# Attention scores of a chunked linear-attention step: two fp32 matmuls of 64 rows in place of three fp32r passes over a block-diagonal operand

## The reference

```python
for t in range(S):
    state = alpha[:, :, t, :, None] * state + np.einsum('bhd,bhe->bhde', k[:, :, t], v[:, :, t])
    y[:, :, t] = np.einsum('bhd,bhde->bhe', q[:, :, t], state)
...
h = np.maximum(xt @ w_tok1, 0.0) @ w_tok2          # token mixer, xt is x transposed
u = x + h.transpose(0, 2, 1)
h2 = np.maximum(u @ w_ch1, 0.0) @ w_ch2            # channel mixer, result u + h2
...
k = np.maximum(xk @ w_k, 0.0); v = k * k @ w_v     # channel mix
r = 1.0 / (1.0 + np.exp(-(xr @ w_r)))              # result r * v
```

## Time and profile before

| quantity | value |
|---|---|
| median of three runs | 812.43 us |
| span of the profiled execution | 811.5 us, 0.9 below the median |
| PE / DVE / ACT / POOL busy | 96% / 61% / 41% / 13% of the span |
| attention of batch 0 alone | 8.4 to 59.1 us |
| three passes of the loop | 59.1 to 471.9 us |
| last mixer and channel mix | 471.9 us to the end |

### The profile page before, as it was taken

How to read it: one execution, slowest core, us unless ns; L and a number is a source line. 1 busy time by engine, 2 the same in 40 slices (tenths; PEclk the granted TensorE clock), 3 DMA queues, 4 the chain that set the end, 5 groups by cost and what they waited for, 6 DMA issues and landing times.

```text
span 811.5 us, 14781 instructions
## 1 busy us (share of the span) xinstructions
PE 779.0 (96%) x4864; PEld 765.0 (94%) x4864; DVE 492.4 (61%) x1463; ACT 332.8 (41%) x848; POOL 103.9 (13%) x146
## 2 busy tenths in 40 slices
PE   6998999999999999899999999999699999999998
PEld 5887999998899999899999999999699999999998
DVE  7987777872677776367787522224835744744751
ACT  4773434331333433143334213125445644743741
POOL 2564000201000110100020013003200000000000
PEclk9999999999999999999999999999899999999999
DMA  9973223330132232112232003200101101101000
GB/s 189 202 171 64 40 42 52 66 57 21 40 51 40 41 69 40 41 30 40 48 50 74 1 30 99 93 30 16 45 29 50 39 29 49 39 29 49 10 29 29
DMA packets 114895, 43.88 MB, mean 54 GB/s; under 512 B 102160, under 2 KB 112016, under 8 KB 114832
## 3 DMA queue, kind: packets, MB, share of 16 engines
q1 hardware_dynamic: 113680, 38.36, 22.8%
q0 software_dynamic: 1152, 4.72, 1.6%
HBM read 33.63 MB, written 9.44 MB: 53 GB/s over the span
## 4 chain that ended last, share of the span: by engine, by line
PE 81%; DVE 8%; issue 5%; ACT 3%; POOL 1%; SPq 1%; DMA 1%; DVEq 0%; ACTq 0%; POOLq 0%
PE bank L633 17%; PE bank L617 17%; PE bank L699 12%; PE bank L677 12%; PE bank L686 5%; PE bank L538 3%; PE bank L522 3%; PE bank L597 3%; PE bank L500 2%; PE bank L603 2%; PE bank L541 2%; PE bank L571 2%; PE bank L544 1%; ACT qs_hi L756 1%; DVE decay L893 1%
## 5 line engine op out<-in xcount | busy, mean ns | idle before, releaser
L756 ACT ACTIVATE qs_hi<-qd,rlast 64x128 fp32r<-64x128 f32 x144 | 57.6, 400 | 145.2 <-DVE qd L903 143.4
L969 DVE SCALAR_TENSOR_TENSOR hid_lo<-bank,hid_hi 128x384 fp32r<-128x384 f32 x96 | 53.1, 553 | 71.4 <-ACT hid_hi L765 71.4
L765 ACT ACTIVATE hid_hi<-bank 128x384 fp32r<-128x384 f32 x96 | 46.5, 485 | 71.7 <-PE bank L617 71.7
L912 DVE SCALAR_TENSOR_TENSOR qs_lo<-qd,rlast,qs_hi 64x128 fp32r<-64x128 f32 x144 | 57.3, 398 | 27.9 <-ACT qs_hi L756 25.6
L845 ACT ACTIVATE relu_k<-bank 128x384 f32<-128x384 f32 x64 | 31.5, 492 | 102.3 <-PE bank L677 77.4
L617 PE MATMUL bank<-u_hi,wch_hi 128*128 128x384 f32 x288 | 71.1, 355 | 0.0
L617 PE MATMUL bank<-u_lo,wch_hi 128*128 128x384 f32 x288 | 66.0, 336 | 0.0
L617 PE MATMUL bank<-u_hi,wch_lo 128*128 128x384 f32 x288 | 65.6, 335 | 0.0
L633 PE MATMUL bank<-hid_lo,wch_hi 128*128 128x384 f32 x288 | 65.5, 334 | 0.0
L633 PE MATMUL bank<-hid_hi,wch_hi 128*128 128x384 f32 x288 | 65.4, 334 | 0.0
L633 PE MATMUL bank<-hid_hi,wch_lo 128*128 128x384 f32 x288 | 65.4, 334 | 0.0
(11 more groups left out here) (126 smaller groups left out, 1855.5 us busy)
## 6 DMA issues: line engine op xcount, KB each, us to landing
w_raw<-in_moe_w_ch SPq DMA_DIRECT2D x12, 384.0 KB, 4.1
x_scratch<-x_half POOLq DMA_DIRECT2D x8, 576.0 KB, 3.5
out<-x_half SPq DMA_DIRECT2D x24, 192.0 KB, 1.9
vt<-in_v SPq DMA_DIRECT2D x44, 96.0 KB, 2.4
qka<-in_q SPq DMA_DIRECT2D x21, 192.0 KB, 3.2
qka<-in_k SPq DMA_DIRECT2D x21, 192.0 KB, 4.0
qka<-in_alpha SPq DMA_DIRECT2D x21, 192.0 KB, 4.2
qka<-x_scratch SPq DMA_DIRECT2D x4, 577.5 KB, 3.9
```

Source lines behind the costliest of these rows:

```text
L756: nc.scalar.activation(dst[lanes, h * P:(h + 1) * P], qd[lanes, i % 4, :], ACT.Copy, scale=rlast[lanes, i % 4:i % 4 + 1])\
L765: nc.scalar.activation(dst, b_ring[t % 2][:, 0:HT], func).then_inc(tile_hi, 1)
L912: nc.vector.scalar_tensor_tensor(qs[1][lanes, cols], qd[lanes, i % 4, :], rlast[lanes, i % 4:i % 4 + 1], qs[0][lanes, cols], ALU.mult, ALU ...
L969: ins = nc.vector.scalar_tensor_tensor(dst, src, 0.0, hi, ALU.max, ALU.subtract)
```

## The change

Scaled q is no longer spread: ACT writes one 128x128 fp32 tile `qs` (`scale_q`), and the scores are two fp32 matmuls, head 0 on partitions 0 to 63 and head 1 on 64 to 127, 128 columns each, each into a PSUM bank of its own (1 and 2; 6 and 7 for odd steps of the first batch). The split of q and k (`split_low`, `ks_hi`) is gone, and so are the zeroing of the block-diagonal tiles and four constants. Since head 1's scores now lie in the bank of `y`, `attention_scores` also waits for `xlo_ready` of the step before (two before in the first batch). `mixer_part` is cut in two, `mixer_front` and `mixer_back`, and a slot of the loop becomes scores, transposes, front, out, back, with lags (0, 1, 1). In slots 1 to 3 front and back are one `token_down` each. The first batch keeps its lags, but its slot is reordered on PE, ACT and DVE.

```diff
@@ -100,9 +100,8 @@
         rlast = sb("rlast", [P, 4])
         qd = sb("qd", [P, 4, P])
 
-        qs = [sb(f"qs_{n}", [P, 2 * P], F32R) for n in ("hi", "lo")]
-        kd = sb("kd", [P, 2, P])
-        ks = [sb(f"ks_{n}", [P, P], F32R) for n in ("hi", "lo")]
+        qs = sb("qs", [P, 4, P])
+        kd = sb("kd", [P, 4, P])
         relu_k = sb("relu_k", [P, 2, HT])
         am = relu_k[:, :, 0:2 * P]
         kdt = relu_k[:, :, 2 * P:3 * P]
...
+        b_tr0 = ps("bank0", 1)
+        b_pair0 = ps("bank12", 2)
+        b_mid = [ps(f"bank{n}", 1) for n in (3, 4, 5)]
+        b_pair1 = ps("bank67", 2)
+        bank = [b_tr0[:, :], b_pair0[:, 0:512], b_pair0[:, 512:1024], *(b[:, :] for b in b_mid),
+                b_pair1[:, 0:512], b_pair1[:, 512:1024]]
         b_ring = [bank[3], bank[4]]
         b_acc = [bank[5], bank[6], bank[7]]
 
+        def second_set(r, i):
+
+            return is_first(r) and i % 2 == 1
+
         def transposed_qka(r, i):
 
-            b_tr = bank[5] if is_first(r) and i % 2 else bank[0]
+            b_tr = bank[5] if second_set(r, i) else bank[0]
             return b_tr[:, 0:P], b_tr[:, P:2 * P], b_tr[:, 2 * P:3 * P]
 
-        def scores_kdT(r, i):
-
-            b_sc = bank[7] if is_first(r) and i % 2 else bank[1]
-            return b_sc[:, 0:2 * P], b_sc[:, 2 * P:3 * P]
+        def scores_both(r, i):
+
+            b_sc = b_pair1 if second_set(r, i) else b_pair0
+            return b_sc[:, :].rearrange("p (h c) -> p h c", h=2)[:, :, 2 * P:3 * P]
+
+        def scores_of(r, i, h):
+
+            return bank[6 + h if second_set(r, i) else 1 + h][:, 2 * P:3 * P]
+
+        def kdT_of(r, i):
+
+            return bank[6 if second_set(r, i) else 1][:, 0:P]
 
         def y_kv(r, i):
 
-            b_y = bank[6] if is_first(r) and i % 2 else bank[2]
+            b_y = bank[7 if second_set(r, i) else 2]
             return b_y[:, 0:W2], b_y[:, P:P + W2]
 
 
...
@@ -250,8 +266,7 @@
 
         def steps_of(r, s):
 
-
-            lags = (0, 2, 3) if is_first(r) else (0, 1, 2)
+            lags = (0, 2, 3) if is_first(r) else (0, 1, 1)
             return [s - n if 0 <= s - n < STEPS else None for n in lags]
 
         def chunk_buffer(r, c):
...
@@ -507,19 +522,16 @@
                 banks = 2 if is_first(r) else 1
                 if not is_first(r) or i >= banks:
                     pe.wait_ge(am_ready, STEPS * r + i + 1 - banks)
+                    pe.wait_ge(xlo_ready, STEPS * r + i + 1 - banks)
                 if i >= banks:
                     pe.wait_ge(kdt_ready, NST * r + min(i + 1 - banks, NST))
-                scores, kdT = scores_kdT(r, i)
                 if c < NC - 1:
-                    nc.tensor.transpose(kdT, kd[:, i % 2, :], ident[:, :])
-                pe.wait_ge(qbd_ready, 2 * (STEPS * r + i + 1))
-                if is_first(r):
-
-                    mm = nc.tensor.matmul(scores, kd[:, i % 2, :], qbd[:, i % 2, :], start=True, stop=True)
-                else:
-                    pe.wait_ge(split_ready, 3 * (STEPS * (r - 1) + i + 1))
-                    for n, (a, b) in enumerate(PASSES):
-                        mm = nc.tensor.matmul(scores, ks[a][:, :], qs[b][:, :], start=(n == 0), stop=(n == 2))
+                    nc.tensor.transpose(kdT_of(r, i), kd[:, i % 4, :], ident[:, :])
+                pe.wait_ge(qs_ready, STEPS * r + i + 1)
+                for h in range(2):
+                    lanes = slice(h * DP, (h + 1) * DP)
+                    mm = nc.tensor.matmul(scores_of(r, i, h), kd[lanes, i % 4, :], qs[lanes, i % 4, :],
+                                          start=True, stop=True)
                 mm.then_inc(scores_done, 1)
...
-            def attention_part(r, s):
-                tr, sc, yo = steps_of(r, s)
-                if not is_first(r) and yo is not None:
-                    attention_out(r, yo)
+            def first_attention(s):
+                tr, sc, yo = steps_of(0, s)
+                if tr is not None:
+                    transposes(0, tr)
+                if yo is not None:
+                    attention_out(0, yo)
                 if sc is not None:
-                    attention_scores(r, sc)
-                if tr is not None:
-                    transposes(r, tr)
-                if is_first(r) and yo is not None:
-                    attention_out(r, yo)
+                    attention_scores(0, sc)
...
-            def mixer_part(b, s):
-                if s < KT:
-                    if s == 0:
-                        token_up(b, 1)
+            def mixer_front(b, s):
+                if s == 0:
+                    token_up(b, 1)
                 elif s < FIRST_UNIT:
                     pe.wait_ge(w_lo_ready, TOK2_END)
-                    for m in range(KC):
-                        token_down(b, s - KT, m)
+                    token_down(b, *divmod(2 * s - 2, KC))
                 else:
                     if s == FIRST_UNIT:
                         pe.wait_ge(w_lo_ready, CH1_END)
                     channel_up(b, s - FIRST_UNIT)
-                    if s > FIRST_UNIT:
-                        channel_down(b, s - FIRST_UNIT - 1)
+
+            def mixer_back(b, s):
+                if 0 < s < FIRST_UNIT:
+                    token_down(b, *divmod(2 * s - 1, KC))
+                elif s > FIRST_UNIT:
+                    channel_down(b, s - FIRST_UNIT - 1)
...
             with pe.Fori(1, B) as r:
-                attention_part(r, 0)
-                mixer_part(r - 1, 0)
-                for s in range(1, SLOTS):
-                    mixer_part(r - 1, s)
-                    attention_part(r, s)
+                for s in range(SLOTS):
+                    tr, sc, yo = steps_of(r, s)
+                    if sc is not None:
+                        attention_scores(r, sc)
+                    if tr is not None:
+                        transposes(r, tr)
+                    mixer_front(r - 1, s)
+                    if yo is not None:
+                        attention_out(r, yo)
+                    mixer_back(r - 1, s)
                 token_up(r, 0)
                 channel_down(r - 1, UNITS - 1)
...
-            def spread_q(r, i):
+                nc.scalar.activation(kdt[:, i % 2, :], kdT_of(r, i), ACT.Copy).then_inc(kdt_ready, 1)
+
+            def scale_q(r, i):
                 act.wait_ge(qd_ready, STEPS * r + i + 1)
-                for h in range(2):
-                    lanes = slice(h * DP, (h + 1) * DP)
-                    dst = qbd[:, i % 2, :] if is_first(r) else qs[0]
-                    nc.scalar.activation(dst[lanes, h * P:(h + 1) * P], qd[lanes, i % 4, :], ACT.Copy,
-                                         scale=rlast[lanes, i % 4:i % 4 + 1])\
-                        .then_inc(qbd_ready, 1)
-                if not is_first(r):
-                    act.wait_ge(kd_ready, STEPS * r + i + 1)
-                    nc.scalar.activation(ks[0][:, :], kd[:, i % 2, :], ACT.Copy).then_inc(ks_hi_ready, 1)
+                nc.scalar.activation(qs[:, i % 4, :], qd[:, i % 4, :], ACT.Copy, scale=rlast[:, i % 4:i % 4 + 1])\
+                    .then_inc(qs_ready, 1)
...
-                dve.wait_ge(qbd_ready, 2 * (STEPS * r + i + 1))
-                for h in range(2):
-                    lanes, cols = slice(h * DP, (h + 1) * DP), slice(h * P, (h + 1) * P)
-                    nc.vector.scalar_tensor_tensor(qs[1][lanes, cols], qd[lanes, i % 4, :],
-                                                   rlast[lanes, i % 4:i % 4 + 1], qs[0][lanes, cols],
-                                                   ALU.mult, ALU.subtract).then_inc(split_ready, 1)
-                dve.wait_ge(ks_hi_ready, STEPS * (r - 1) + i + 1)
-                nc.vector.tensor_tensor(ks[1][:, :], kd[:, i % 2, :], ks[0][:, :], ALU.subtract)\
-                    .then_inc(split_ready, 1)
+                nc.vector.tensor_tensor(kd[:, i % 4, :], kT, suffix[:, i % 2, :], ALU.mult).then_inc(kd_ready, 1)
 
             def mask(r, i):
                 dve.wait_ge(consts_g, 15)
                 dve.wait_ge(scores_done, STEPS * r + i + 1)
-                nc.vector.copy_predicated(am[:, i % 2, :], causal[:, :].bitcast(U32),
-                                            scores_kdT(r, i)[0])\
-                    .then_inc(am_ready, 1)
+                nc.vector.copy_predicated(am[:, i % 2, :].rearrange("p (h t) -> p h t", h=2),
+                                          causal[:, :].bitcast(U32).rearrange("p (h t) -> p h t", h=2),
+                                          scores_both(r, i)).then_inc(am_ready, 1)
 
             def outputs(r, i):
                 c, p = step(i)
...
+                                          scores_both(r, i)).then_inc(am_ready, 1)
 
             def outputs(r, i):
                 c, p = step(i)
@@ -943,24 +956,15 @@
                 xs = slice(p * W2, (p + 1) * W2)
                 nc.vector.tensor_tensor(x[1][:, c, xs], y_ps, x[0][:, c, xs], ALU.subtract).then_inc(xlo_ready, 1)
 
```

(109 more changed lines are left out.)

83 lines of the change are left out of this document (44 added, 39 removed).

## The result

The changed kernel takes **837.98 us** (828.68 to 838.99, four runs), the kernel before 812.03 (810.9 to 812.52, four runs beside them): 1.0294 times as long over all of these runs (so not the quotient of the medians), 95% interval 1.0244 to 1.0345. The forecast was 804.0 with a range up to 828. The profiled run took 837.91 us; its span is 836.3, 24.8 more than before. The run of 828.68 had a granted clock of 0.996 on average instead of 0.992; there is no trace of it. One execution of experiment 9 took 1541.87 us, nearly twice the other three, and is left out of its times.

A forecast was written before the change was run, and what follows sets the result against it. DVE was taken to bound the first batch and PE the three passes, with some 25 us of waits and lowered clock. Span 811.5 + 10.5 - 17.5 - 1.4 = 803.1, with 0.9 to the median 804.0; range 795 to 828.

The forecast's parts named there:

- Scores on PE: Loop, 72 steps: two half-height fp32 matmuls take 0.34 us instead of 0.36, height changes free; -1.4 us.
- rival C: Loop scores: both heads overlap fully, 0.22 us per pair, 8.6 us less, 795.4; chance 0.10.
- rival B: Loop scores: switching height empties the array, 0.32 us per step, 23 us more, 827.0; chance 0.27 with smaller switches.
- First batch: Reordered first-batch slot: each step waits on a chain through three engines; +10.5 us, bounds zero and 13.
- The circle: First batch: mask, out, x_hi, outputs, next mask take 2.57 us per step against DVE's 2.03.
- Loop's waits: Three passes: of some 25 us of waits and lowered clock 6.5 stay; -18.3, taken as -17.5 us.
- The new wait at slot 4: Loop, slot 4: scores of step 4 wait for x_lo of step 3; 1.2 us each pass, 3.6 in all.
- A: Loop scores: records run one after another without overlap, 0.45 us, 7.9 us more, 811.9; chance 0.22.
- D: First batch does not get longer, so the sum lacks 10.5 us: 793.5; chance 0.04.
- The mark: Time from line 533's first record to line 515's: 0.34 us forecast, 0.45 A, over 0.6 rival B, 0.22 rival C.
- the turning point: Loop scores: the result turns when the score pair costs 0.46 us, a switch of 0.06.

The follow-up runs named there:

- experiment 9: Changed kernel plus three unused full-height fp32r matmuls of 384 columns in slots 3 to 13 of the first batch: 832.1 to 834.7 us, ratio 1.0241.
- experiment 2: Changed kernel with both score matmuls over all 128 rows, all else as changed: 821.08 us.
- experiment 3: Changed kernel with both score matmuls on the same 64 rows (head 0 twice), so they cannot overlap: 861.59 us, one run.
- experiment 4: Changed kernel with the transpose kdT moved between the two heads' score matmuls: 882.83 us, one run.
- experiment 8: Kernel of experiment 7 with the changed kernel's first-batch order and four buffers of kd and spread q, banks of before: 816.17 us.
- experiment 7: Kernel before with new loop slots, no split, all scores one block-diagonal fp32 matmul; first batch and banks kept: 803.22 us, ratio 0.9884.
- Experiment 10: Kernel before with only the split dropped, loop scores one fp32 matmul; slots, banks and first batch kept: 802.08 us, ratio 0.9867.
- (6): Kernel before with the loop's new slot order alone, the split kept and placed directly behind scale_qk: 811.21 us, ratio 0.9979.

## Why the prediction was wrong

**Scores on PE, forecast -1.4 us: the step that failed.** It said "Nothing is charged for going from full-height to half-height matmuls", judged by a change between turned and plain operands. Experiments 2, 3 and 4 show 0.17 us for each change of height, two a step, 72 steps in the loop: +24. That PE empties there fits this price, but the runs show the price alone. Against that the heads overlap in full, not by half: rival C was right on it, 0.22 for the pair and not 0.34. Per slot, 0.335 for the changes less 0.14 (0.36 to 0.22) is +0.195 of the measured +0.25. The other 0.05 stands in experiment 2 as well (4.93 against 4.795 - 0.36 + 0.45 = 4.885), so it isn't the height. Most of it lies in `channel_down`: 1.60 us here and in experiment 2, where line 633 took 1.56. In the new slot it follows out and no longer `channel_up`, and its second record starts 0.260 behind its first instead of 0.173. Why is open. In all +18 us where -1.4 stood.

This is rival B's mechanism with its price (0.16 forecast, 0.17 measured). Its 827.0 was counted on three record times and on the loop alone; it lacked what follows. I had given it 0.27 because no row had the case, and took the nearest seamless row as evidence, which it was not. TensorEngine Tiling (the Trainium skill), section Key Properties, states that a change of tiling mode drains the engine and that different tiles work in parallel; both now have their numbers here, 0.17 us and 6 ns between starts. TensorE: Matmul & The Clock Gate (the Trainium skill), section Single matmul latency, puts the drain of a single bf16 matmul at about 175 ns. Taken as the price of one change, an estimate from that page's figure and not something it states, two would cost 0.35 a step, near the 0.335 measured for these fp32 ones.

**First batch, forecast +10.5, measured +22.2.** The circle was right: 2.57, and chunks 1 to 4 cost 16 x 0.54 = 8.6 in experiment 8 as forecast. Two parts were mis-sized or missing. With full-height scores the new order costs 13.0 to 13.2 (experiment 8), which is already the upper bound of 13 that the prediction gave for the term. Its first steps up to 21 us come 3.4 later and not 1.3: the first mask comes at 10.85 instead of 9.85, and the low clock of the start lasts 6.2 longer than in experiment 7. How much of the 3.4 is the order and how much the clock wasn't separated. The rest, 81.32 - 73.00 = 8.3, comes under the low clock. Up to 21 us the two kernels are alike (the mask of step 3 at 20.88 and 20.87), and behind 42 us the masks are 2.57 apart in both kernels, so at full clock the changes of height don't lengthen the circle, but mask 9 comes at 42.40 instead of 36.14 (6.3, under the half clock up to 40.9), and the last mask and the batch's end, in the low stretch from 75.1 on, add 2.0. In the stretch before 40.9 PE is busy 7.00 of 7.00 us (the window of 27 to 34 above), so the changes of height are paid there as well: from `kdT` to the first score record 0.351 us, where experiment 8 has 0.213 at the same clock. How the 6.3 divides between clock and heights wasn't measured. The prediction named the clock only as something that comes back in the loop. Experiment 9 gives 5.6 of the 8.3 back, with the half clock ended early. Why the clock rises so late with half-height scores (40.9, against 21.0 with full height and 18.1 with the filler) the runs show only as a fact; the cause wasn't isolated.

**Loop's waits, forecast -17.5: right in kind, some 2 off.** The three passes are 2.9 longer and hold 18 of the scores' term, so about 15 came back. The new wait at slot 4 is there, as drawn (waits of PE in the loop of the kernel after):

```profile
PE bank L529 <- DVE x_lo L957: 4.1, 3, 1.4
PE bank L515 <- issue: 1.5, 2, 0.9
PE bank L529 <- DVE kd L930: 0.9, 2, 0.6
```

4.1 in three against 3.6 forecast, and the clock no longer falls behind the heads. Experiment 10 shows that the dropped split earns this gain without the new slots: -10.3 net of 72 x 0.1 for the longer matmul. The slot reordering, which I credited with its share, is worth -0.2% at best (6) and +1.1 us beside experiment 10 (7).

**Rivals A and D** are out: the records of two heads don't queue, and the first batch did get longer. The mark that I set for them was ill drawn: from the first score record to the transposes are 0.43 us, near A's 0.45 and far from B's "over 0.6". Read alone it would have said A; B's other half stands ahead of line 533, and only the equal starts and experiment 3 tell the two apart.

The three terms again, measured: scores +18 (forecast -1.4), first batch +22.2 (+10.5), waits -15 (-17.5), the rest -0.3: 24.9 against the span's 24.8. The -15 is what is left of the passes once the scores' term is taken out, so that the sum closes proves nothing about how the two divide.

## What to carry to other kernels

A matmul over half the rows of the array is not a cheaper matmul of the same stream. Count its switches: two per island, 0.17 us each here, more than it saves over padding with zeros (0.46 for the block-diagonal fp32 matmul; 0.22 + 0.335 = 0.555 for the pair with both its changes). By these numbers it would begin to pay with two pairs in a row (0.44 + 0.335 = 0.78 against 0.92); that is an estimate, and no run here has the case.

When a case isn't in the trace, the nearest row that differs in kind (turned operands) is no bound for it (another height). Put the full cost of the mechanism into the sum if the turning point is small; here 0.06 us a switch decided the sign.

If a change needs more banks, ask what it shares them with: with this sharing the old order of the first batch was worse still, and the new one cost 13 us, more than the 10.3 that the dropped split earned. The part that earned, the dropped split, needed none of it.

## What the runs showed of the hardware that was not expected

- Matmuls on the two row halves of the array, into different banks, overlap fully: records of two heads start 6 ns apart, and four last 0.49 us where two last 0.48 (experiment 4's single head).
- PE can be busy in the records for 20 us on end (7.00 of 7.00 us in the window shown and in those on either side, 20 to 41) and still be granted half its clock, up to 40.9 us; with unused full-height matmuls in 11 slots it was full from 18.1. The granted clock that the profile prints says 1.00 where its first record has not come yet; the spacing of equal records (0.43 for two against 0.22) tells the level. The section Seeing it yourself of TensorE: Matmul & The Clock Gate (the Trainium skill) warns that clock events in a trace are not fully reliable; what this case adds is a record that is missing at the start, not one that is wrong.
- A stage can get shorter when PE gets more to do: in experiment 9's trace the first batch ends 5.6 us sooner. Three of its runs are 3 to 6 us below the changed kernel's median, but not below its fastest run.
